# The first units of an attention stage: stacked operands of head 0 copied by engines, loads on two queues, the scale folded into a split, eight PSUM banks

## The chip, the core and the metric

The kernel runs on one core of a Trainium2 chip. The metric is the device time of one execution in microseconds (us). The engines are TensorE (PE, with its weight loads PEld), VectorE (DVE), ScalarE (ACT), GpSimd (POOL) and SyncE (SP). SP does no arithmetic; it issues DMA transfers, and so can ACT. SBUF is the on-chip memory of 128 partitions, PSUM the accumulator memory of eight banks.

## What is computed

```python
def _attn_ref(q, k, v, proj):            # 2 x 8 heads, 768 rows, 64 columns; proj 64 x 6
    scale = 1.0 / np.sqrt(D)
    q_bits = (einsum('bhsd,dk->bhsk', q, proj) > 0); k_bits = (... k ...)
    mask = q_bucket[..., :, None] == k_bucket[..., None, :]     # the six bits as one number
    scores = np.where(mask, scale * np.matmul(q, k.transpose(0, 1, 3, 2)), -1e9)
    attn = softmax over the last axis (denominator + 1e-9)
    return attn @ v
def reference(...):
    x = attention output as 1536 rows x 512
    x = _moe_ref(x, ...)      # router with noise, 2 of 8 experts, 512 -> 1024 -> 512, relu
    return _moe2_ref(x, ...)  # 512 -> 2048 -> 512 with h * sigmoid(1.702 h)
```

## The kernel before

The kernel is written engine by engine; each engine's program is a list in its own order, and semaphores order the engines among each other. Attention comes first, then the router, the experts and the last layer.

Attention works on 8 pairs of heads (PAIRS) and, for each head, on 6 blocks of 128 query rows; one block of one head is a step n, 96 steps in all. A step n is: `scores(n)` on TensorE into a psS bank pair, `statistics(n)` on VectorE (row maximum, and from it exp_arg), `exponentials(n)` on ACT, `transposes(n)` on TensorE into psT, `evac(n)` on ACT. The loop runs scores two steps ahead. `weighted` and `back` form the product with v for the head before.

A score is one product of stacked operands. A head's slot in W holds four tiles of 128 rows by 768 columns, QA, QB, KA and KB. QA is q_hi over q_hi, KA is k_hi over k_lo; QB is q_lo over the query's hash bits, and KB is k_hi over the key's hash bits. q_hi and q_lo are the two parts into which a float32 number is split for the fast product type (fp32r). So QA'KA + QB'KB gives the score and a large term that marks whether the hash bits agree.

A pair is prepared in eight units. Units 0 to 3 transpose q (0, 1) and k (2, 3), half of the columns each, for both heads at once (head 0 in partitions 0 to 63, head 1 in 64 to 127). ACT then copies the transposed half from PSUM into q_hi or k_hi, and VectorE subtracts it to form q_lo or k_lo. Units 4 to 7 multiply q and k by the hash matrices hash_m, and VectorE turns the result into bits (L938, one operation for each head and unit), which it writes straight into rows 64 to 127 of QB and KB. The remaining 12 pieces of 64 rows (6 of them q, 6 k) are moved from q_hi, q_lo, k_hi, k_lo into the slots by DMA from SP's queue (L420). For pair 0 all eight units run ahead of the first scores and use the four psS banks (`unit_bank`); for later pairs unit u of pair pr + 1 goes with step u of pair pr and uses psM.

The factor 1/8 is applied by POOL to the loaded q (L486) before the transposes; TensorE's unit 0 waits for it (`s_scaled`). POOL's list between two pairs also has `split_chunk(0, pr)`, which splits one of the first expert's weight chunks (L478, L480) once it has been staged:

```python
for pr in range(PAIRS):
    pool.wait_ge(s_q, 32 * (pr + 1))
    nc.gpsimd.tensor_scalar(q_raw[:], q_raw[:], SCALE, None, ALU.mult).then_inc(s_scaled, 1)
    if pr < 4:
        split_chunk(0, pr)
```

SP's list: q and k of pair 0 (L370), proj, the router's weights and the noise (L405 to L409); then for each pair the 12 stack moves, q and k of the next pair, v of this pair (L375), and a weight chunk (L381). VectorE first builds hash_m from proj (L907 to L920).

## Time and profile before

| what | value |
|---|---|
| median of 3 runs | 972.48 us (972.25 to 973.07) |
| the profiled execution: its own time | 973.35 us |
| its span in the trace | 971.6 us |
| TensorE busy | 893.4 us, 92% of the span |
| VectorE, ACT, POOL busy | 401.8, 402.5, 314.8 us |
| mean granted TensorE clock | 0.97 of full speed |
| attention, 0 to 302 us | TensorE busy 260.9 us |

Times in the trace are microseconds from the start of the span. Busy time is the time in which an engine had an instruction in work; the chain of waits is followed back from the last instruction, at each step to what released it. A granted clock of 1.00 is 2.4 GHz and 0.50 is 1.2 GHz. PEld, the weight load, overlaps PE.

### The profile page before, as it was taken

To read this page: it belongs to the slowest core of one execution; us is meant where nothing else is said; L and a number is where in the kernel's file an instruction comes from. 1 tells how busy PE (TensorE), PEld (TensorE's weight loads), DVE (VectorE), ACT (ScalarE), POOL (GpSimd) and SP (SyncE) were. 2 spreads that over 40 slices of the span, in tenths; PEclk is the share of its full clock that TensorE was granted. 3 is DMA by queue.
4 is the path that set the end of the run, shared out by engine and by line. 5 is a ranking of instruction groups with operands and counts; after the bars stand their busy time and mean duration, and the time that the engine had idled before them with its cause. 6 is when DMAs were issued, how large, how long until landed. Compare 5 with 4: busy or idle time off the path is not lost.

```text
span 971.6 us, 13442 instructions
## 1 busy us (share of the span) xinstructions
PE 893.4 (92%) x4964; PEld 779.9 (80%) x4964; DVE 401.8 (41%) x746; ACT 402.5 (41%) x687; POOL 314.8 (32%) x199
## 2 busy tenths in 40 slices
PE   3699999999998799999999999993699999999997
PEld 2566676666665689999999999993699999999996
DVE  4577767766774612222222222211443333333322
ACT  1566676676674124343343343411222322332222
POOL 1222020000240135564655656597970010000000
PEclk8899999999999789999999999998799999999999
DMA  7445624642423123655546456455331010000000
GB/s 161 112 115 152 163 71 104 168 115 57 110 89 109 29 64 124 184 160 177 165 158 192 161 163 196 147 181 170 127 95 38 32 43 22 32 0 0 33 1 32
DMA packets 66778, 103.34 MB, mean 106 GB/s; under 512 B 31676, under 2 KB 33724, under 8 KB 66716
## 3 DMA queue, kind: packets, MB, share of 16 engines
q1 hardware_dynamic: 55216, 76.65, 27.9%
q0 software_dynamic: 4480, 13.11, 4.5%
q10 hardware_dynamic: 7020, 12.78, 3.7%
q8 instruction: 36, 0.59, 0.3%
q14 instruction: 26, 0.21, 0.1%
HBM read 64.57 MB, written 19.07 MB: 86 GB/s over the span
## 4 chain that ended last, share of the span: by engine, by line
PE 82%; DVE 8%; issue 3%; ACT 2%; DMA 2%; SPq 2%; POOL 1%; ACTq 0%; DVEq 0%; POOLq 0%
PE psS L770 15%; PE psS L869 14%; PE psS L884 9%; PE psS L788 7%; PE psV L656 6%; PE psT L642 5%; PE psS L631 5%; PE psV L884 5%; PE psV L788 4%; PE psM L788 4%; DVE W L938 2%; PE psM L618 2%; PE psT L801 1%; ACT probT L1240 1%; PE psM L613 1%
## 5 line engine op out<-in xcount | busy, mean ns | idle before, releaser
L480 POOL TENSOR_TENSOR W<-staged,W 128x1024 fp32r<-128x1024 f32 x80 | 191.8, 2401 | 122.8 <-ACT W L1300 117.6
L770 PE MATMUL psS<-xT_hi,W 128*128 128x416 f32 x512 | 142.2, 359 | 1.1 <-DVE xT_lo L1113 1.1
L869 PE MATMUL psS<-x2T_hi,W 128*128 (+1 forms) x512 | 134.5, 344 | 1.6 <-DVE x2T_lo L1180 1.6
L1231 ACT ACTIVATE prob<-psS,exp_arg 128x768 f32<-128x768 f32 x96 | 95.5, 994 | 37.2 <-DVE exp_arg L947 37.1
L944 DVE TENSOR_REDUCE neg_max<-psS 128x1 f32<-128x768 f32 x96 | 91.5, 953 | 45.8 <-PE psS L631 44.9
L631 PE MATMUL psS<-W 128*128 128x384 f32 x384 | 93.8, 367 | 11.4 <-DMA W<-k_hi 9.4
L1240 ACT ACTIVATE probT<-psT 128x768 f32<-128x768 f32 x96 | 78.0, 812 | 57.8 <-PE psT L642 56.1
L869 PEld LDWEIGHTS psS<-x2T_hi,W 128*128 128x128 f32 x512 | 95.1, 192 | 6.8 <-issue 2.0
L1119 DVE SCALAR_TENSOR_TENSOR hT_lo<-psS,hT_hi 128x416 fp32r<-128x416 f32 x64 | 37.9, 591 | 149.5 <-ACT hT_hi L1293 132.0
L631 PEld LDWEIGHTS psS<-W 128*128 128x128 f32 x384 | 65.1, 194 | 38.6 <-issue 34.2
L770 PEld LDWEIGHTS psS<-xT_hi,W 128*128 128x128 f32 x512 | 92.7, 188 | 2.2 <-issue 1.2
L1187 DVE TENSOR_TENSOR g_sb<-psS,sig 128x384 f32<-128x384 f32 x64 | 35.7, 557 | 138.5 <-ACT sig L1374 138.5
L1374 ACT ACTIVATE sig<-psS 128x384 f32<-128x384 f32 x64 | 31.4, 491 | 146.0 <-PE psS L869 146.0
L770 PE MATMUL psS<-xT_lo,W 128*128 128x416 f32 x256 | 89.9, 351 | 0.0
L478 POOL TENSOR_TENSOR W<-staged,ones_col 128x1024 fp32r<-128x1024 f32 x24 | 45.8, 1909 | 134.5 <-DMA staged<-in_moe_w 96.0
L869 PE MATMUL psS<-x2T_lo,W 128*128 (+1 forms) x256 | 87.6, 342 | 0.0
L642 PE MATMUL psT<-ident,prob 128*128 128x128 f32 x576 | 80.0, 275 | 5.6 <-ACT probT L1240 5.6
L884 PE MATMUL psS<-W,g_hi 128*128 128x512 f32 x256 | 79.9, 393 | 1.7 <-issue 1.7
L642 PEld LDWEIGHTS psT<-ident,prob 128*128 128x128 f32 x576 | 66.8, 142 | 16.3 <-issue 13.1
L1300 ACT ACTIVATE W<-staged 128x1024 fp32r<-128x1024 f32 x56 | 59.1, 1055 | 30.6 <-DVE x_sb L1134 21.1
L788 PE MATMUL psS<-hT_hi,W 128*128 128x416 f32 x256 | 69.4, 352 | 0.0
L656 PE MATMUL psV<-probT,v_raw 128*64 128x384 f32 x360 | 68.0, 499 | 0.0
(221 smaller groups left out, 1397.4 us busy)
## 6 DMA issues: line engine op xcount, KB each, us to landing
staged<-in_moe_w SPq DMA_DIRECT2D x64, 512.0 KB
ys_dram<-x_sb ACTq DMA_DIRECT2D x60, 208.0 KB
W<-q_hi SPq DMA_DIRECT2D x32, 192.0 KB, 3.3
W<-k_hi SPq DMA_DIRECT2D x32, 192.0 KB, 3.7
staged<-in_moe_w_in SPq DMA_DIRECT2D x8, 512.0 KB
staged<-in_moe_w_out SPq DMA_DIRECT2D x8, 512.0 KB
q_raw<-in_q SPq DMA_DIRECT2D x16, 192.0 KB, 4.0
k_raw<-in_k SPq DMA_DIRECT2D x16, 192.0 KB, 4.2
```

The costliest lines, as they stand in the source:

```text
L480: nc.gpsimd.tensor_tensor(W[:, at + BLOCK:at + BLOCK + CH], staged[:, n % 2], W[:, at:at + CH].bitcast(F32), ALU.subtract).then_inc(s_spli ...
L631: last = nc.tensor.matmul(psS[:, n % 2, half, 0:HALF], stack(slot, a)[:, qt * P:(qt + 1) * P], stack(slot, b_)[:, half * HALF:(half + 1) * ...
L642: last = nc.tensor.transpose(psT[:, half, j * P:(j + 1) * P], prob[:, n % 2, c * P:(c + 1) * P], ident[:])
L656: last = nc.tensor.matmul(av_bank(hd)[half * D:(half + 1) * D, 0:HALF], v_raw[:, hd // 2 % 2, hd % 2, c * D:(c + 1) * D], probT[:, hd % 2, ...
L770: mm = nc.tensor.matmul(psS[:, 0, f % 2, 0:TM], W[:, at:at + P], x[:, t % 2, c], start=c == 0 and n == 0, stop=c == DC - 1 and n == 2)
L788: mm = nc.tensor.matmul(y_bank[d][:, 0:TM], W[:, at:at + P], h[:, f % 2], start=f == 0 and n == 0, stop=f == FC - 1 and n == 2)
L869: mm = nc.tensor.matmul(psS[:, 0, f % 2, 0:GN], W[:, at:at + P], x[:, bass.ds(buf + c * GN, GN)], start=c == 0 and n == 0, stop=c == DC - ...
L884: mm = nc.tensor.matmul(out_bank[j], gp[:, f % 2, j * P:(j + 1) * P], W[:, at:at + DM], start=f == 0 and n == 0, stop=f == GC - 1 and n == 2)
L944: nc.vector.tensor_reduce(neg_max[:, o, 0:1], psS[:, o, :, 0:HALF], mybir.AxisListType.XY, ALU.max, negate=True).then_inc(s_stat, 1)
L1231: nc.scalar.activation(prob[:, o, :].rearrange("p (a c) -> p a c", a=2), psS[:, o, :, 0:HALF], ACT.Exp, bias=exp_arg[:, o, 0:1], scale=exp ...
L1240: nc.scalar.activation(probT[:, hd % 2, :, t * P:(t + 1) * P].rearrange("p (a c) q -> p a c q", a=2), psT[:, :, 0:HALF].rearrange("p a (c ...
L1300: A(W[:, at:at + CH], staged[:, n % 2], ACT.Copy).then_inc(s_whi, 1)
```

## The change

For pair 0 alone, head 0's six stack pieces are written by engines in place of DMA: POOL copies q_hi twice into QA, VectorE copies q_lo into QB, ACT copies k_hi into KA and KB and k_lo into KA. Head 1's six pieces stay with SP, and `moved(pr)` counts the moves that are due (48 for pair 0, 96 for each later pair). `s_first` counts the six copies; `s_thr` counts the four threshold operations of head 0, which VectorE does first; those of head 1 follow between the first statistics. `scores(0)` waits for `s_first` and `s_thr` only, `scores(6)` for head 1's moves, and `transposes(0)` for all eight units, since units 4 to 7 of pair 0 now use psT, psV and psM.

The second head's q and k of pair 0 and the second half of proj are loaded from ACT's queue. SP loads q and k of pair 1 directly behind proj, ahead of the stack moves, and the router's weights and the noise behind v. POOL's scaling of q is gone for all pairs: ACT's q_hi is formed with scale 1/8 and VectorE's q_lo as PSUM times 1/8 minus q_hi. TensorE runs six products of ident with itself into psM before unit 0 (`unread(6)`), whose result nobody reads.

```diff
--- before.py
+++ after.py
@@ -216,7 +216,11 @@
 
         def unit_bank(u, first):
 
-            return psS[:, u // 2 % 2, u % 2] if first else psM
+            return (psS[:, 0, 0], psS[:, 0, 1], psS[:, 1, 0], psS[:, 1, 1], psT[:, 0], psT[:, 1], psV, psM)[u] if first else psM
+
+        def moved(pr):
+
+            return max(96 * pr - 48, 0)
 
         def columns(t, buf, j):
 
@@ -253,7 +257,8 @@
         s_den = sem("s_den")
         s_oT = sem("s_oT")
         s_back = sem("s_back")
-        s_scaled = sem("s_scaled")
+        s_first = sem("s_first")
+        s_thr = sem("s_thr")
         s_norm = sem("s_norm")
         s_x = sem("s_x")
 
@@ -355,8 +360,10 @@
             eng.wait_ge(s_exp, STEPS)
             eng.wait_ge(s_bias, STEPS)
             eng.wait_ge(s_back, HEADS)
-            eng.wait_ge(s_stq, 96 * PAIRS)
-            eng.wait_ge(s_stk, 96 * PAIRS)
+            eng.wait_ge(s_stq, moved(PAIRS))
+            eng.wait_ge(s_stk, moved(PAIRS))
+            eng.wait_ge(s_first, 6)
+            eng.wait_ge(s_thr, 4)
             eng.wait_ge(s_norm, HEADS)
 
         @block.sync
@@ -401,26 +408,30 @@
                     sp.wait_ge(s_osplit, 8 * (t - E + 1))
                     stage_over(t + 1, used)
 
-            load_qk(0)
+            sp.dma_start(q_raw[:, :, 0], q_v[0].rearrange("p (t d) -> p t d", d=D)).then_inc(s_q, 16)
+            sp.dma_start(k_raw[:, :, 0], k_v[0].rearrange("p (t d) -> p t d", d=D)).then_inc(s_k, 16)
             sp.dma_start(proj_sb[0:D, :], proj).then_inc(s_proj, 16)
-            sp.dma_start(proj_sb[D:P, :], proj).then_inc(s_proj, 16)
-            sp.dma_start(w_router[:, :, 0:E], w_gate.rearrange("(c p) e -> p c e", p=P)).then_inc(s_wr, 16)
-            sp.dma_start(w_router[:, :, E:2 * E], w_noise.rearrange("(c p) e -> p c e", p=P)).then_inc(s_wr, 16)
-            sp.dma_start(noise_sb[:].rearrange("p (b t) e -> p b (t e)", b=B),
-                         noise.rearrange("(b p t) e -> p b (t e)", b=B, t=NT)).then_inc(s_wr, 16)
+            load_qk(1)
             for pr in range(PAIRS):
                 if pr >= 2:
                     sp.wait_ge(s_S, PS * (pr - 1))
                 for hi, lo, s, u in ((q_hi, q_lo, s_stq, 2), (k_hi, k_lo, s_stk, 4)):
                     sp.wait_ge(s_ud, UNITS * pr + u)
-                    for hh in range(2):
+                    for hh in range(0 if pr else 1, 2):
                         rows, slot = slice(hh * D, (hh + 1) * D), 2 * (pr % 2) + hh
                         moves = (((QA, 0, hi), (QA, 1, hi), (QB, 0, lo)), ((KA, 0, hi), (KA, 1, lo), (KB, 0, hi)))[u // 2 - 1]
                         for which, at, src in moves:
                             sp.dma_start(stack(slot, which)[at * D:(at + 1) * D].bitcast(F32), src[rows].bitcast(F32)).then_inc(s, 16)
-                if pr + 1 < PAIRS:
+                if pr == 0:
+                    load_v(0)
+                    sp.dma_start(w_router[:, :, 0:E], w_gate.rearrange("(c p) e -> p c e", p=P)).then_inc(s_wr, 16)
+                    sp.dma_start(w_router[:, :, E:2 * E], w_noise.rearrange("(c p) e -> p c e", p=P)).then_inc(s_wr, 16)
+                    sp.dma_start(noise_sb[:].rearrange("p (b t) e -> p b (t e)", b=B),
+                                 noise.rearrange("(b p t) e -> p b (t e)", b=B, t=NT)).then_inc(s_wr, 16)
+                elif pr + 1 < PAIRS:
                     load_qk(pr + 1)
-                load_v(pr)
+                if pr:
+                    load_v(pr)
                 if pr < 6:
                     stage_chunk(0, pr)
             for c in range(6, 8):
@@ -481,11 +492,12 @@
                                         ALU.subtract).then_inc(s_split, 1)
 
             pool.wait_ge(s_const, 16)
-            for pr in range(PAIRS):
-                pool.wait_ge(s_q, 32 * (pr + 1))
-                nc.gpsimd.tensor_scalar(q_raw[:], q_raw[:], SCALE, None, ALU.mult).then_inc(s_scaled, 1)
-                if pr < 4:
-                    split_chunk(0, pr)
+            pool.wait_ge(s_hi, 2)
+            for which, at in ((QA, 0), (QA, 1)):
+                nc.gpsimd.tensor_scalar(stack(0, which)[at * D:(at + 1) * D], q_hi[0:D], 1.0, None, ALU.mult).then_inc(s_first, 1)
+            pool.wait_ge(s_first, 6)
+            for c in range(4):
+                split_chunk(0, c)
             pool.wait_ge(s_S, PS * (PAIRS - 1))
             for c in range(4, 8):
                 split_chunk(0, c)
@@ -595,15 +607,15 @@
             def unit(pr, u, first=False):
 
                 if u == 0:
-                    pe.wait_ge(s_scaled, pr + 1)
+                    pe.wait_ge(s_q, 32 * (pr + 1))
                 if u == 2:
                     pe.wait_ge(s_k, 32 * (pr + 1))
                 if u == 4 and first:
                     pe.wait_ge(s_hash, 18)
                 if not first:
                     pe.wait_ge(s_ud, UNITS * pr + u)
-                elif u >= 4:
-                    pe.wait_ge(s_ud, u - 3)
+                elif u in (4, 6):
+                    pe.wait_ge(s_ud, u - 2)
                 side, half = (u // 2) % 2, u % 2
                 ps = unit_bank(u, first)
                 if u < 4:
@@ -621,10 +633,13 @@
             def scores(n):
 
                 slot, qt = (n // NT) % 4, n % NT
-                if n % PS == 0:
+                if n == 0:
+                    pe.wait_ge(s_thr, 4)
+                    pe.wait_ge(s_first, 6)
+                elif n == NT or n % PS == 0:
                     pe.wait_ge(s_ud, UNITS * (n // PS + 1))
-                    pe.wait_ge(s_stq, 96 * (n // PS + 1))
-                    pe.wait_ge(s_stk, 96 * (n // PS + 1))
+                    pe.wait_ge(s_stq, moved(n // PS + 1))
+                    pe.wait_ge(s_stk, moved(n // PS + 1))
                 at_least(pe, s_exp, n - 1)
                 for i, (a, b_) in enumerate(((QA, KA), (QB, KB))):
                     for half in range(2):
@@ -636,6 +651,8 @@
             def transposes(n):
                 pe.wait_ge(s_exp, n + 1)
                 at_least(pe, s_evA, n)
+                if n == 0:
+                    pe.wait_ge(s_ud, UNITS)
                 for half in range(2):
                     for j in range(NT // 2):
                         c = half * (NT // 2) + j
@@ -665,7 +682,13 @@
                     last = nc.tensor.transpose(av_bank(hd)[:, j * P:(j + 1) * P], oT(hd)[:, j * P:(j + 1) * P], ident[:])
                 last.then_inc(s_back, 1)
 
+            def unread(n):
+
+                for i in range(n):
+                    nc.tensor.matmul(psM[:, 0:P], ident[:], ident[:], start=True, stop=True)
+
             pe.wait_ge(s_const, 8)
+            unread(6)
             for u in range(UNITS):
                 unit(0, u, True)
             for n in range(2):
@@ -919,13 +942,16 @@
                         nc.vector.tensor_scalar(hash_m[rows, side, m, cols[0]], src[rows], size, None, ALU.mult).then_inc(s_hash, 1)
                         nc.vector.tensor_scalar(hash_m[rows, side, m, cols[1]], src[rows], -size, None, ALU.mult).then_inc(s_hash, 1)
 
-            def unit(pr, u, first=False):
+            def unit(pr, u, first=False, heads=(0, 1)):
                 ps = unit_bank(u, first)
                 if u < 4:
                     c = slice((u % 2) * HALF, (u % 2 + 1) * HALF)
                     dve.wait_ge(s_hi, 4 * pr + u + 1)
                     hi, lo = ((q_hi, q_lo), (k_hi, k_lo))[u // 2]
-                    last = nc.vector.tensor_tensor(lo[:, c], ps[:, 0:HALF], hi[:, c].bitcast(F32), ALU.subtract)
+                    if u < 2:
+                        last = nc.vector.scalar_tensor_tensor(lo[:, c], ps[:, 0:HALF], SCALE, hi[:, c].bitcast(F32), ALU.mult, ALU.subtract)
+                    else:
+                        last = nc.vector.tensor_tensor(lo[:, c], ps[:, 0:HALF], hi[:, c].bitcast(F32), ALU.subtract)
                 else:
                     side, half = (u // 2) % 2, u % 2
                     c = slice(half * HALF, (half + 1) * HALF)
@@ -933,10 +959,10 @@
                     if u == 4:
                         at_least(dve, s_S, PS * (pr - 1))
                     t, s, w = ((thrQ, sclQ, QB), (thrK, sclK, KB))[side]
-                    for hh in range(2):
+                    for hh in heads:
                         rows = slice(hh * D, (hh + 1) * D)
                         last = nc.vector.tensor_scalar(stack(2 * (pr % 2) + hh, w)[D:P, c], ps[rows, 0:HALF], t[rows], s[rows], ALU.is_gt, ALU.mult)
-                last.then_inc(s_ud, 1)
+                last.then_inc(s_ud if 1 in heads else s_thr, 1)
 
             def statistics(n):
                 o = n % 2
@@ -965,10 +991,17 @@
                                         row_rec[:, hd % 2].rearrange("p (a j) -> p a j", a=2)[:, :, :, None].to_broadcast([P, 2, NT // 2, D]),
                                         ALU.mult).then_inc(s_norm, 1)
 
-            for u in range(UNITS):
+            for u in range(4):
                 unit(0, u, True)
+                if u == 1:
+                    dve.wait_ge(s_ud, 2)
+                    nc.vector.tensor_copy(stack(0, QB)[0:D], q_lo[0:D].bitcast(F32)).then_inc(s_first, 1)
+            for u in range(4, UNITS):
+                unit(0, u, True, (0,))
             for n in range(2):
                 statistics(n)
+                for u in (2 * n + 4, 2 * n + 5):
+                    unit(0, u, True, (1,))
             for n in range(STEPS):
                 hd, t = divmod(n, NT)
                 if t == 0 and hd >= 2:
@@ -1221,8 +1254,10 @@
                 c = slice((u % 2) * HALF, (u % 2 + 1) * HALF)
                 act.wait_ge(s_unit, UNITS * pr + u + 1)
                 if u in (0, 2) and not first:
-                    act.wait_ge((s_stq, s_stk)[u // 2], 96 * pr)
-                nc.scalar.activation((q_hi, k_hi)[u // 2][:, c], unit_bank(u, first)[:, 0:HALF], ACT.Copy).then_inc(s_hi, 1)
+                    act.wait_ge((s_stq, s_stk)[u // 2], moved(pr))
+                    act.wait_ge(s_first, 6)
+                nc.scalar.activation((q_hi, k_hi)[u // 2][:, c], unit_bank(u, first)[:, 0:HALF], ACT.Copy,
+                                     scale=SCALE if u < 2 else 1.0).then_inc(s_hi, 1)
 
             def exponentials(n):
                 o = n % 2
@@ -1240,8 +1275,15 @@
                 nc.scalar.activation(probT[:, hd % 2, :, t * P:(t + 1) * P].rearrange("p (a c) q -> p a c q", a=2),
                                      psT[:, :, 0:HALF].rearrange("p a (c q) -> p a c q", q=P), ACT.Copy).then_inc(s_evA, 1)
 
+            act.dma_start(q_raw[:, :, 1], q_v[1].rearrange("p (t d) -> p t d", d=D)).then_inc(s_q, 16)
+            act.dma_start(k_raw[:, :, 1], k_v[1].rearrange("p (t d) -> p t d", d=D)).then_inc(s_k, 16)
+            act.dma_start(proj_sb[D:P, :], proj).then_inc(s_proj, 16)
             for u in range(4):
                 unit(0, u, True)
+            act.wait_ge(s_hi, 4)
+            for which, at, src, done in ((KA, 0, k_hi, 0), (KB, 0, k_hi, 0), (KA, 1, k_lo, 4)):
+                at_least(act, s_ud, done)
+                nc.scalar.activation(stack(0, which)[at * D:(at + 1) * D], src[0:D].bitcast(F32), ACT.Copy).then_inc(s_first, 1)
             exponentials(0)
             for n in range(STEPS):
                 if n + 1 < STEPS:
```

## Rows read from the trace of the kernel before

**Rows 1.** The page's chain that ended last: shares of the span by engine.

```profile
PE 82%; DVE 8%; issue 3%; ACT 2%; DMA 2%; SPq 2%; POOL 1%; ACTq 0%; DVEq 0%; POOLq 0%
```

**Rows 2.** Table of stages: length, then each engine's busy us, clock, DMA share, GB/s.

```profile
0.00:302.00 302.00, 260.86 (x1584) 187.01 (x1584) 202.54 (x370) 186.64 (x321) 53.36 (x44) 0.97 0.45 114
302.00:345.00 43.00, 34.75 (x202) 30.08 (x203) 24.73 (x93) 12.68 (x22) 6.50 (x15) 0.82 0.24 82
```

**Rows 3.** Chain of waits, first 60 us: start, length, what.

```profile
18.37 0.67 SPq L420
...
23.66 4.52 DMA staged<-in_moe_w
...
28.25 1.90 POOL W L478
...
30.23 2.34 POOL W L480
32.56 2.10 POOL q_raw L486
...
34.71 0.90 PE psM L613 x3
```

**Rows 4.** Timeline, first 50 us: start, length, engine, line, operation.

```profile
0.82 1.28 ACT L1225 ACT_TABLE_LOAD   x1 [0.82 <-PEq L1418]
...
5.26 2.16 POOL L486 TENSOR_SCALAR q_raw<-q_raw 128x768 f32<-128x768 f32 x1 [1.63 <-DMA q_raw<-in_q]
...
6.90 0.55 DVE L907 CAST proj_hi<-proj_sb 128x6 fp32r<-128x6 f32 x1 [6.90 <-DMA proj_sb<-in_proj]
...
7.57 1.51 PE L613 MATMUL psS<-ident,q_raw 128*128 128x128 f32 x6 [7.57 <-POOL q_raw L486]
...
9.11 1.08 DVE L928 TENSOR_TENSOR q_lo<-psS,q_hi 128x384 fp32r<-128x384 f32 x2
9.12 0.49 ACT L1225 ACTIVATE q_hi<-psS 128x384 fp32r<-128x384 f32 x1
...
11.51 5.58 DVE L938 TENSOR_SCALAR W<-psS,thr 64x384 fp32r<-64x384 f32 x8
...
22.60 2.90 PE L631 MATMUL psS<-W 128*128 128x384 f32 x8 [9.38 <-DMA W<-k_hi]
...
24.26 0.96 DVE L944 TENSOR_REDUCE neg_max<-psS 128x1 f32<-128x768 f32 x1 [7.17 <-PE psS L631]
25.25 0.16 DVE L947 SCALAR_TENSOR_TENSOR exp_arg<-neg_max 128x2 f32<-128x2 f32 x1
...
27.39 0.82 PE L642 MATMUL psT<-ident,prob 128*128 128x128 f32 x6
...
35.65 0.49 ACT L1225 ACTIVATE q_hi<-psM 128x384 fp32r<-128x384 f32 x1 [6.59 <-PE psM L613]
...
36.69 1.48 PE L642 MATMUL psT<-ident,prob 128*128 128x128 f32 x6
...
42.68 0.97 PE L631 MATMUL psS<-W 128*128 128x384 f32 x4
```

**Rows 5.** Short stretches: columns as in rows 2, after the length.

```profile
4.50:5.00 0.50, 0.00 (x0) 0.00 (x0) 0.00 (x0) 0.00 (x0) 0.00 (x0) 1.00 1.26 284
...
34.00:35.00 1.00, 0.29 (x2) 0.29 (x3) 0.00 (x0) 0.00 (x0) 0.66 (x1) 0.50 0.00 0
```

**Rows 6.** DMA issues of the first 8 us: KB each, median us to landing.

```profile
q_raw<-in_q SPq DMA_DIRECT2D x2, 192.0 KB, 3.3
k_raw<-in_k SPq DMA_DIRECT2D x2, 192.0 KB, 3.5
...
proj_sb<-in_proj SPq DMA_DIRECT2D x2, 1.5 KB, 2.5
```

**Rows 7.** Timeline of a weight chunk's split.

```profile
61.03 2.13 DVE L947 SCALAR_TENSOR_TENSOR exp_arg<-neg_max 128x2 f32<-128x2 f32 x1
```

**Rows 8.** Groups of VectorE, 0 to 310: count, busy us, mean ns.

```profile
L947 DVE SCALAR_TENSOR_TENSOR exp_arg<-neg_max 128x2 f32<-128x2 f32 x96 | 26.3, 274 | 3.3
```

## The prediction

> **What bounds the kernel now.** I began with the page. Its chain of waits runs through TensorE for 82% of the span [rows 1], so a change pays only where TensorE stands still. The table of stages gives attention 302 us, with TensorE busy for 260.9 of them, and the routing stage behind it 43 us [rows 2]. The diff touches the first unit of work of head 0, the q scaling in front of every pair, and nothing past attention; so I read attention's first 43 us.
>
> The chain of waits [rows 3] shows two holes. First: SP issues the twelve stack transfers one after another; the last issue ends at 19.04 (18.37 + 0.67) and the first score product starts at 22.60 [rows 4]. TensorE stood still for 9.4 us before it. Second: after the first transposes of probabilities (27.39 + 0.82 = 28.2) TensorE stands still until 34.71 [rows 3, 4]. It waits for pair 1's q to be scaled by POOL, and POOL sits in program order behind weight chunk 0, whose transfer lands at 28.2, plus 1.90 and 2.34 us of split and 2.10 us of scaling [rows 3]. The reader is to see that the second hole hangs on SP's queue too: chunk 0 is issued behind all stack transfers, pair 1's q and k, and v. From 35.65, where ACT evacuates the first q unit of pair 1 [rows 4], the steps follow one another without such holes. So I use the start of that q_hi, 35.65, as the milestone: behind it both kernels have the same order of work, and what the milestone gains the end gains, unless something takes it back.
>
> **The change, part by part, up to the first scores.**
>
> *Loads on two queues.* Landing takes 3.3 us for q, 3.5 for k, 2.5 for proj [rows 6]. The queues begin at 0.8, as ACT's table load does [rows 4]; q was landed when POOL took it at 5.26. With the second half issued beside the first, q lands at 0.8 + 3.3 = 4.1 at the earliest. If ACT's first issue stands behind its table load (0.82, 1.28 us [rows 4]) it lands near 2.1 + 3.3 = 5.4. I take 4.7. The DMA engines are already full at 284 GB/s in 4.5 to 5.0 [rows 5], and the four loads are 768 KB, so k cannot land much before 5.5, and proj, behind it, lands near 5.8 instead of 6.8. The six products of unread() start once ident is there and are six transposes long, 1.5 us at the pace of the first ones [rows 4]; they end before q lands and cost nothing. With a q that landed at once they would cost up to 1.5.
>
> *No scaling by POOL before the transposes.* POOL's 2.16 us (5.26 to 7.42 [rows 4]) leaves the path. From the first q transpose to the end of the second q_hi took 9.12 + 0.49 - 7.57 = 2.04 us, so both q_hi halves stand at 4.7 + 2.1 = 6.8. The factor inside the split is one more operand of an operation of 384 columns: nothing, on ACT and on DVE. At worst it is 0.05 us each.
>
> *VectorE becomes the path.* It builds the hash matrices: 6.90 to 9.11 now, of which the first cast took 0.55 us and ended at 7.45, as POOL's scaling ended (7.42) [rows 4]; a small one takes 0.16, so it lost about 0.4. From 5.8 that is 1.8 us: done at 7.6. Then q_lo, two for 1.08; the new copy of q_lo, 64 rows by 768; k_lo, 1.1; and four threshold operations of head 0 alone, where eight took 5.58, so 2.8. The copy is not in the trace: a reduction over 768 columns takes 0.96 [rows 4], a small operation like exp_arg 0.16 [rows 4], and I take 0.6. Sum 1.1 + 0.6 + 1.1 + 2.8 + 0.15 of handovers = 5.75, so scores could start at 13.4.
>
> *POOL's new copies against VectorE.* POOL copies q_hi twice, 64 rows by 768. Its scaling of 768 columns took 2.16; I take that for each, so POOL is busy about 4.3 us from 6.8, before score operands are due. But the first cast above waited for POOL's end, and an exp_arg of 0.16 us took 2.13 us while POOL split a chunk [rows 7]. VectorE's hash operations (5.8 to 7.6) and its q_lo copy read and write SBUF like that cast. They can lose from nothing to 4.3 us, the first scores then starting at 13.4 or 17.7. The two meet for certain, by these times, and half of the work would be caught: I take 2.2, scores at 15.6. The Trainium skill ("SBUF — State Buffer", Who interferes with whom) says the pair of ports is locked for a whole instruction, and that whichever of the two engines issues first blocks the other. By it the bound is one POOL copy caught at a time: 15.5 if one catches VectorE, 17.7 if both do; the cast's row agrees.
>
> *Copies on ACT.* Three of 768 columns; q_hi of 384 takes 0.49 [rows 4], so 0.98 each. Two run behind k_hi (near 8.5 to 10.4) and the third behind k_lo, beside the 2.8 us of thresholds. Cost nothing; without that cover 1.
>
> *Twelve stack transfers less six.* Head 0 needs none. Head 1's six are issued between roughly 10 and 18 and land, at the 4.5 us of the weight chunk [rows 3], by 22.5. Its first scores are step 6, now at 42.68 [rows 4], then at about 32: hidden.
>
> **From the first scores to the milestone.** Scores to first reduction takes 24.26 - 22.60 = 1.66. VectorE then does statistics (0.96 + 0.16 + handovers, 1.2), two thresholds of head 1 (1.4), statistics (1.2), two thresholds (1.4): 5.2. This is a wait that before had not: the transposes of step 0 now write psT, from which unit 5's thresholds are read last, and wait for all eight units. Queued behind them are pair 1's first unit, and ACT's evacuation. Then transposes take 0.82, or 1.48 at the lower clock (0.50 granted in 34 to 35 [rows 5]), and unit 0 of pair 1 to q_hi 0.94 (35.65 - 34.71), or about 0.65 at the higher. The whole is 9.3 at the low and about 7.7 at the high one. TensorE is idle for under 3 us here instead of 6.5; I take 8.6. The milestone: 15.6 + 8.6 = 24.2, against 35.65: 11.4 us.
>
> The second hole is thereby gone: POOL no longer stands between q and its transposes. Pair 1's q and k are issued once the first transposes are done, about 6.3 to 9, and landed long before 22. What is late next is VectorE, not a transfer.
>
> **What takes some back.** Weight chunk 0 is split now in the hole, 28.25 to 32.56, where nobody cares. Afterwards its transfer, issued near 17 to 20, lands 4.5 us later [rows 3], and the 4.2 us of split falls on steps 0 to 2. An exp_arg caught loses up to 1.97 [rows 7]; two can be caught, and some of it lies under ACT's other work. I charge 0.7 (0 to 4). The seven later scalings on POOL cost the path nothing, since no transpose waited for them; their going gives nothing. The same chunks 1 to 7 meet the same steps, shifted; their collisions may change by 1 each way.
>
> Sum: 973.35 (the profiled execution, span 971.6) - 11.4 + 0.7 = 962.7. It lies 0.9 above the median of the runs, 972.48; so 961.8.
>
> Bounds. Best: scores at 13.4, milestone 7.7 later, nothing taken back: 35.65 - 21.1 = 14.6, time 957.9. Worst: 17.7 and 9.3, 4 taken back: 35.65 - 27.0 - 4 = 4.6, time 967.8. Not all bad ends meet, so 957.5 to 966.5.
>
> **Rivals.**
>
> *Part of the gain goes to the lock between VectorE and POOL.* Both copies catch VectorE fully and chunk 0 catches two exp_args that all count: the worst above, 965 to 968. For it: rows 7 and the cast. Against: ACT's work covers some of it.
>
> *Slower: the lock in the steps.* All exp_args together lost 26.3 - 96 x 0.16 = 10.9 us to it [rows 8], at most about 2 each. The eight chunks bring 16 POOL operations; if every one caught one exp_arg fully, each losing the length of its split less 0.16 [rows 3, 4], that is 8 x 1.7 + 8 x 2.2 = 31 us, 20 more than now, and 973.35 - 11.4 + 20 - 0.9 = 981. It decides from six more full catches on. Against: chunks 4 to 7 are released by a step's scores, so they meet the same exp_args as now.
>
> *Same: the transfers give it back.* If head 1's operands landed only when they are needed today (42.7), 11 us late for the new step 6, nothing would be left: 972.5. For it: they now share the DMA engines with pair 1's loads. Against: 20 us of room.
>
> *More than the sum.* VectorE is not caught, and TensorE keeps its clock: the best above, 956 to 958.
>
> **How the numbers follow.** The forecast (957.5 to 965) 0.76; most lost to the lock (965 to 970.5) 0.13; more than the sum 0.05; given back 0.03; slower 0.03. A measurement here can tell 0.2%, 1.9 us. The first three are faster: 0.94; same 0.03; slower 0.03.
>
> **What would show it.** The first score product near 15.6, and no DMA in front of it but VectorE's threshold. Transposes of step 0 released by VectorE near 22 to 23; ACT's first q_hi from psM near 24. No wait of TensorE for q_raw or POOL. VectorE's hash operations or its q_lo copy far longer than 0.16 and 0.6 while POOL copies: the lock, and how much. Exp_arg near 2 us in steps 0 to 3. Attention's end near 291. Wrong it would be if ACT's loads came late by its table load beyond 1.3 us, if POOL's copies take far over 2.2 us each, or if a later stage holds work that waits for a time and not for a step.

## The result, and the profile after

The changed kernel takes 961.05 us (median of 4 runs, 959.97 to 961.26), against 972.78 for the kernel before: ratio 0.9872, 95% interval 0.9855 to 0.989. The forecast was 961.8, between 957.5 and 966.5. The profiled execution takes 960.99 with a span of 959.1, so 12.4 and 12.5 us less than that of before. By the medians it is 972.78 - 961.05 = 11.7 us.

The page's chain and the table of stages of the changed kernel, to be held against [rows 1, 2]:

```profile
PE 83%; DVE 9%; issue 3%; ACT 2%; DMA 2%; POOL 1%; SPq 0%; ACTq 0%; DVEq 0%; POOLq 0%
```

```profile
0.00:290.00 290.00, 262.92 (x1599) 188.04 (x1600) 204.81 (x371) 188.70 (x324) 41.35 (x40) 0.99 0.46 115
```

Attention is over some 12.5 us earlier. The timeline of its first 30 us (start, length, engine, line, operation, and in brackets the idle time before it and its releaser), against [rows 4]:

```profile
2.24 2.93 PE L688 MATMUL psM<-ident 128*128 128x128 f32 x12 [2.24 <-POOL ident L469]
...
4.96 1.49 PE L625 MATMUL psS<-ident,q_raw 128*128 128x128 f32 x6
...
6.59 0.17 DVE L930 CAST proj_hi<-proj_sb 128x6 fp32r<-128x6 f32 x1 [6.59 <-DMA proj_sb<-in_proj]
...
7.15 4.62 POOL L497 TENSOR_SCALAR W<-q_hi 64x768 fp32r<-64x768 f32 x2 [3.53 <-ACT q_hi L1259]
...
7.22 0.80 DVE L943 TENSOR_SCALAR hash_m<-proj_hi 64x6 fp32r<-64x6 f32 x1
...
8.56 0.80 DVE L943 TENSOR_SCALAR hash_m<-proj_hi 64x6 fp32r<-64x6 f32 x1
...
9.48 1.02 DVE L952 SCALAR_TENSOR_TENSOR q_lo<-psS,q_hi 128x384 fp32r<-128x384 f32 x2
...
10.54 0.55 DVE L998 CAST W<-q_lo 64x768 fp32r<-64x768 f32 x1
...
12.95 0.67 DVE L964 TENSOR_SCALAR W<-psT,thr 64x384 fp32r<-64x384 f32 x1 [0.22 <-PE psT L630]
...
13.91 0.67 DVE L964 TENSOR_SCALAR W<-psV,thr 64x384 fp32r<-64x384 f32 x1 [0.29 <-PE psV L630]
...
14.51 0.66 DVE L964 TENSOR_SCALAR W<-psM,thr 64x384 fp32r<-64x384 f32 x1
...
15.22 1.67 PE L646 MATMUL psS<-W 128*128 128x384 f32 x8 [0.78 <-DVE W L964]
...
21.35 1.51 PE L659 MATMUL psT<-ident,prob 128*128 128x128 f32 x6 [1.83 <-DVE W L964]
22.06 1.89 POOL L489 TENSOR_TENSOR W<-staged,ones_col 128x1024 fp32r<-128x1024 f32 x1 [10.28 <-DMA staged<-in_moe_w]
22.23 1.73 DVE L973 SCALAR_TENSOR_TENSOR exp_arg<-neg_max 128x2 f32<-128x2 f32 x1
...
23.61 0.48 ACT L1259 ACTIVATE q_hi<-psM 128x384 fp32r<-128x384 f32 x1
...
25.58 0.85 DVE L973 SCALAR_TENSOR_TENSOR exp_arg<-neg_max 128x2 f32<-128x2 f32 x1
...
27.60 0.97 PE L646 MATMUL psS<-W 128*128 128x384 f32 x4
```

The reader is to see four things. The scores start at 15.22 in place of 22.60, released by VectorE's threshold (the bracket) and no longer by a transfer. The transposes of step 0 wait for VectorE at 21.35. The first q_hi of pair 1 starts at 23.61 in place of 35.65, 12.04 earlier, and nothing waits for POOL there. And VectorE is caught: hash operations of 0.16 us take 0.80 while POOL copies, exp_arg takes 1.73 and 0.85 while POOL splits chunk 0 (0.16 otherwise).

Where the gain stands as the steps go on is read from the starts of ACT's evacuations (L1240 before, L1275 after), which both kernels have in the same order. The table gives how many us earlier than in the kernel before each of them starts, for the changed kernel, for a second profile of the same kernel, and for the experiments below.

| kernel | q_hi of pair 1 | step 4 | step 32 | step 36 | step 92 |
|---|---|---|---|---|---|
| changed | 12.04 | 13.03 | 13.24 | 12.56 | 12.64 |
| changed, again | 11.10 | 11.55 | 11.55 | 11.57 | 11.66 |
| scale in the split alone | 5.66 | 5.84 | 6.36 | 6.07 | 6.11 |
| head 0 by DMA | 4.43 | 4.74 | 5.20 | 5.05 | 5.02 |
| all loads on SP | 10.93 | 11.36 | 11.83 | 11.85 | 11.87 |
| no unread | 11.38 | 12.26 | 12.75 | 12.78 | 12.76 |
| POOL after the hash matrices | 13.69 | 12.93 | 13.25 | 13.25 | 13.33 |
| split with one input | 12.50 | 11.98 | 12.41 | 12.41 | 12.85 |
| all thresholds first | 10.41 | 11.34 | 11.76 | 11.81 | 11.74 |
| no lock, no-match left out | 12.09 | 12.09 | 12.54 | 12.55 | 13.42 |
| no lock, exact | 12.91 | 14.10 | 14.20 | 14.10 | 14.73 |
| the same, gaps filled | 13.38 | 14.84 | 14.89 | 14.95 | 15.54 |
| the same, gaps idle | 11.40 | 12.86 | 12.70 | 12.75 | 13.58 |

Behind attention the programs are the same, but not their times: from POOL's first gather to the end of the span it is 638.0 us before, 638.2 after, 637.2 in the second profile, and from 635.1 (all loads on SP) to 639.2 (split with one input) in the others. So an edit worth less than 2 us is not read from the whole time, but from this table. Each row is one profile, and the two rows of the changed kernel differ by 0.9 to 1.7 us, so the table doesn't tell differences of that size either, unless the rows of the trace show where they come from.

### The profile page after: what moved, and what is told of

Its sections match the earlier page's. It is cut to its first block, busy times and chain, and to the rows that moved or that the text cites. A ratio compares the mean times of both kernels' runs of the same rounds, so it can differ in the third digit from the quotient of the medians.

```text
span 959.1 us, 13465 instructions
## 1 busy us (share of the span) xinstructions
PE 895.8 (93%) x4976; PEld 780.6 (81%) x4976; DVE 403.6 (42%) x747; ACT 405.0 (42%) x690; POOL 302.7 (32%) x193
## 4 chain that ended last, share of the span: by engine, by line
PE 83%; DVE 9%; issue 3%; ACT 2%; DMA 2%; POOL 1%; SPq 0%; ACTq 0%; DVEq 0%; POOLq 0%
PE psS L793 15%; PE psS L892 14%; PE psS L907 9%; PE psS L811 7%; PE psV L673 6%; PE psS L646 5%; PE psV L907 5%; PE psT L659 5%; PE psV L811 4%; PE psM L811 4%; DVE W L964 3%; PE psM L630 2%; PE psT L824 1%; DVE neg_max L970 1%; ACT probT L1275 1%
## 5 line engine op out<-in xcount | busy, mean ns | idle before, releaser
L1275 ACT ACTIVATE probT<-psT 128x768 f32<-128x768 f32 x96 | 78.0, 812 | 57.5 <-PE psT L659 55.7
L646 PE MATMUL psS<-W 128*128 128x384 f32 x384 | 91.6, 360 | 3.9 <-ACT prob L1266 3.0
```

The costliest lines, as they stand in the source:

```text
L646: last = nc.tensor.matmul(psS[:, n % 2, half, 0:HALF], stack(slot, a)[:, qt * P:(qt + 1) * P], stack(slot, b_)[:, half * HALF:(half + 1) * ...
L1275: nc.scalar.activation(probT[:, hd % 2, :, t * P:(t + 1) * P].rearrange("p (a c) q -> p a c q", a=2), psT[:, :, 0:HALF].rearrange("p a (c ...
```

## The experiments

**1. The second hole alone.** The kernel before, with only the scaling moved.

```diff
-                    pe.wait_ge(s_scaled, pr + 1)
+                    pe.wait_ge(s_q, 32 * (pr + 1))
...
-                pool.wait_ge(s_q, 32 * (pr + 1))
-                nc.gpsimd.tensor_scalar(q_raw[:], q_raw[:], SCALE, None, ALU.mult).then_inc(s_scaled, 1)
```

with ACT's scale and VectorE's factor as in the change. 

> The kernel before, with one part of the change alone: the factor 1/8 inside the split of q, and no scaling by POOL for any pair. Theory (two holes, each removed by its own part): the second hole of 6.5 us goes, since pair 1's transposes wait for the load alone, and the first cast no longer stands behind POOL (0.4); the exp_arg of step 2, held by chunk 0's split until 30.2, now counts, up to 0.8. First scores at 22.2, ACT's first q_hi from psM at 29 to 30 in place of 35.65; 966.5, between 965 and 968. Rival (one chain: the new transposes just wait longer for something else, such as pair 1's q, issued behind the stack moves and landing near 25, or chunk 0's split on VectorE): gain under 4 us, above 968.5.

966.24 us, ratio 0.9912 (0.9892 to 0.9933). First scores at 22.34, q_hi at 29.99. The second hole was worth 6.1 us by itself at step 92, and the rival falls. The whole time fell by more, 8.6 us against the 974.88 that the kernel before took on the same chip; 1.8 of that lies behind attention in the profile (636.2 in place of 638.0), where nothing was edited. So the milestone confirms the theory, and the hit on 966.5 is in part chance.

**2. The first hole put back.** The changed kernel with head 0's pieces moved by SP.

```diff
-            return max(96 * pr - 48, 0)
+            return 96 * pr
...
-                    for hh in range(0 if pr else 1, 2):
+                    for hh in range(2):
...
-            for which, at in ((QA, 0), (QA, 1)):
-                nc.gpsimd.tensor_scalar(stack(0, which)[at * D:(at + 1) * D], q_hi[0:D], 1.0, None, ALU.mult).then_inc(s_first, 1)
```

and the same for VectorE's and ACT's copies; scores(0) waits for the moves. 

> The changed kernel, with head 0's six stack pieces moved by SP's DMA again; all else stays. Theory: the engine copies carry the first hole. SP's twelve moves are issued from 10 to 19 and landed near 22, so scores start near 21.5 to 22.5 in place of 15.2, and ACT's first q_hi from psM comes near 30 in place of 23.6; 967, between 966 and 968.5. Rival (the copies only move the wait: thresholds and statistics on VectorE fill the time either way, since the milestone waits for all eight units): the milestone moves by under 3 us, below 964.

968.87 us, ratio 0.9938 (0.9918 to 0.9958), 0.4 above the expected range, and q_hi at 31.22 where 30 was expected. The timeline of this run:

```profile
6.55 0.17 DVE L926 CAST proj_hi<-proj_sb 128x6 fp32r<-128x6 f32 x1 [6.55 <-DMA proj_sb<-in_proj]
...
8.39 1.02 DVE L948 SCALAR_TENSOR_TENSOR q_lo<-psS,q_hi 128x384 fp32r<-128x384 f32 x2
...
22.18 2.90 PE L642 MATMUL psS<-W 128*128 128x384 f32 x8 [8.74 <-DMA W<-k_hi]
...
28.96 1.51 PE L655 MATMUL psT<-ident,prob 128*128 128x128 f32 x6 [1.16 <-DVE W L960]
...
31.22 0.49 ACT L1251 ACTIVATE q_hi<-psM 128x384 fp32r<-128x384 f32 x1
```

Scores are back at 22.18, and by the table the engine copies are worth 12.64 - 5.02 = 7.6 us, or 6.6 against the second profile. This kernel has everything else of the change and is yet 1.1 slower at step 92 than experiment 1: its transposes of step 0 wait for head 1's thresholds (28.96). So with head 0 moved by DMA the rest of the change (queues, order of loads, banks, thresholds, unread) brings nothing beyond experiment 1 that shows. The engine copies are priced here with the second hole gone; no run has them alone on the kernel before. The run also prices the lock: without POOL's copies the time from the cast to q_lo is 8.39 - 6.55 = 1.84 us, with them 9.48 - 6.59 = 2.89. VectorE lost 1.05. In three other kernels without POOL's copies at that time (experiments 1, 6 and 12) this stretch is 1.84 too.

**3. One queue.** The three loads of ACT's queue moved back to SP's, in the old order.

```diff
-            act.dma_start(q_raw[:, :, 1], q_v[1].rearrange("p (t d) -> p t d", d=D)).then_inc(s_q, 16)
-            act.dma_start(k_raw[:, :, 1], k_v[1].rearrange("p (t d) -> p t d", d=D)).then_inc(s_k, 16)
-            act.dma_start(proj_sb[D:P, :], proj).then_inc(s_proj, 16)
```

> The changed kernel, with all six loads of pair 0 issued by SP again, in the old order. Theory: the second queue saves issue time only, of which the bytes hide part: proj lands near 6.9 in place of 6.5, q near 5.2 in place of 4.8. POOL then starts near 7.5, and its catch of VectorE stays. First scores 0.3 to 0.8 us later, time up by 0.3 to 0.8. Rival (the queues moved nothing, because the DMA engines are full): no change within 0.2. Second rival (proj late and POOL late no longer overlap as now, the catch changes): up by 1 to 2.

961.48 us, ratio 0.9863 (0.9842 to 0.9883). First scores at 15.64, 0.42 later than in the first profile of the changed kernel and 0.16 later than in the second. The transposes of q started at the same time (4.97), and proj came 0.34 and 0.49 later (6.93); but q_lo started only 0.05 and 0.16 later (9.53), since VectorE was held for less while POOL copied. The same program up to the first scores gave them at 14.76 in experiment 7. So what the second queue is worth, under half a microsecond, is lost in the spread, and the run tells neither the theory nor the rival.

**4. No unread products at the start.**

```diff
-            unread(6)
```

> The changed kernel without the six unread products ahead of the first unit. They took 2.93 us in the trace and ended about when q landed. Theory 1: they buy a higher TensorE clock earlier: without them the k transposes and the hash products up to 14.3 run at the lower pace, first scores 0.3 to 0.6 us later, time up by 0.3 to 1. Theory 2: nothing waits for TensorE there, VectorE being the path: no change within 0.3, or down by 0.1.

961.04 us, ratio 0.9858 (0.9838 to 0.9878). First scores at 15.21, as in the changed kernel, and the first transposes at 4.98, released by the load of q, so the unread products hold nothing up; but the eight of them take 2.93 us and not 1.67, and q_hi comes at 24.27. That looked like theory 1, until the kernel was run again.

**5. The changed kernel again.** No edit. 

> The changed kernel again, unaltered, to see what of the differences between runs lies in the chip and not in the edit. Theory (the moment at which TensorE's clock rises again near 24 us is not set by the kernel): first scores at 15.2 and ACT's first q_hi from psM near 23.6 come back within 0.1, but the evacuation of step 4, 31.51 in the first run, comes between 31.5 and 32.6, since two other runs that are the same kernel up to there gave 32.45 and 32.56. Time 960 to 962. Rival (it repeats): 31.5 within 0.1.

961.22 us (960.54 to 964.28), ratio 0.9877 (0.985 to 0.9904). Its timeline, and the stretches of both profiles (length, busy us of PE, PEld, DVE, ACT and POOL, then the granted clock), the first profile first:

```profile
15.48 2.93 PE L646 MATMUL psS<-W 128*128 128x384 f32 x8 [0.77 <-DVE W L964]
...
22.29 1.51 PE L659 MATMUL psT<-ident,prob 128*128 128x128 f32 x6 [1.16 <-DVE W L964]
...
24.55 0.48 ACT L1259 ACTIVATE q_hi<-psM 128x384 fp32r<-128x384 f32 x1
```

```profile
15.00:17.00 2.00, 1.67 (x8) 1.35 (x8) 0.93 (x2) 0.00 (x0) 0.00 (x0) 1.00 0.99 207
17.00:21.00 4.00, 0.97 (x4) 0.65 (x4) 3.83 (x8) 2.16 (x4) 0.00 (x0) 0.96 1.01 244
21.00:26.00 5.00, 4.65 (x26) 4.54 (x26) 4.74 (x6) 2.97 (x7) 3.87 (x2) 0.69 0.05 19
```

```profile
15.00:17.00 2.00, 1.52 (x5) 1.52 (x6) 0.42 (x1) 0.00 (x0) 0.00 (x0) 0.50 1.01 207
17.00:21.00 4.00, 2.92 (x9) 2.04 (x7) 3.67 (x7) 1.22 (x3) 0.00 (x0) 0.50 0.98 241
21.00:26.00 5.00, 3.84 (x17) 3.64 (x17) 3.95 (x6) 3.10 (x6) 3.60 (x2) 0.50 0.04 15
```

The same program got a clock of 1.00 for its first scores once and 0.50 the other time. Six unread products at 2.2 us do not settle that: of the seven profiles that have them and in which TensorE idled for some 0.8 us before the first scores, five got 1.00 (the first, and experiments 6, 7, 9 and 10) and two 0.50 (this one and experiment 3); without them, in one profile, it was 0.50. The step-4 entry differs by 1.5 us between two profiles of one kernel, and at step 92 1.0 is left; 0.7 of it went between steps 32 and 36, where the first profile had an exp_arg of 2.31 us and the second two of 0.63 and 1.27:

```profile
111.02 2.31 DVE L973 SCALAR_TENSOR_TENSOR exp_arg<-neg_max 128x2 f32<-128x2 f32 x1
```

So the kernel does not repeat, and the rival falls. The theory was too narrow: first scores came 0.26 and q_hi 0.94 later, not within 0.1, and step 4 at 32.99, not by 32.6.

**6. POOL's copies later.** One wait more, in POOL's list.

```diff
             pool.wait_ge(s_hi, 2)
+            pool.wait_ge(s_hash, 18)
```

> The changed kernel, with one more wait: POOL starts its two copies of q_hi only when VectorE has built the hash matrices. Theory (the two engines' common lock costs VectorE 1.1 us: hash matrices done at 9.4 in place of 8.3): first scores at 14.1 to 14.3 in place of 15.22, time 1.0 lower, 960. POOL's copies end near 13.1, before the last threshold. Rival (the catch only moves to the q_lo copy, which then wants its 0.55 us inside POOL's first copy): first scores 14.9 or later, gain under 0.4. Second rival (TensorE's earlier start falls into the stretch at the lower clock, 10.7 to 13.6): the first scores come earlier but run at the lower pace, gain 0.4 to 0.7.

960.66 us, ratio 0.9872 (0.9857 to 0.9887).

```profile
8.50 4.37 POOL L498 TENSOR_SCALAR W<-q_hi 64x768 fp32r<-64x768 f32 x2 [4.88 <-DVE hash_m L944]
...
9.38 0.55 DVE L999 CAST W<-q_lo 64x768 fp32r<-64x768 f32 x1
...
13.97 1.67 PE L647 MATMUL psS<-W 128*128 128x384 f32 x8 [0.76 <-DVE W L965]
...
21.96 0.48 ACT L1260 ACTIVATE q_hi<-psM 128x384 fp32r<-128x384 f32 x1
...
24.15 2.37 POOL L491 TENSOR_TENSOR W<-staged,W 128x1024 fp32r<-128x1024 f32 x1
24.17 2.37 DVE L974 SCALAR_TENSOR_TENSOR exp_arg<-neg_max 128x2 f32<-128x2 f32 x1
```

The scores start at 13.97, 1.25 and 1.51 earlier than in the two profiles of the changed kernel (0.79 than in experiment 7, the same program up to there), so the lock's price of 1.05 came back. They ran at the higher pace (1.67), so the second rival falls too. The cast of q_lo took 0.55 inside POOL's first copy: it was not held, and the first rival falls. But the 1.65 won at q_hi (21.96) was gone at step 4: an exp_arg met the second half of chunk 0's split at its first moment and lost 2.2. What remained at step 92 is 13.33, against 12.64 and 11.66.

**7. The chunk's first half with one input.**

```diff
-                    nc.gpsimd.tensor_tensor(W[:, at:at + CH], staged[:, n % 2], ones_col[:].to_broadcast([P, CH]), ALU.mult).then_inc(s_whi, 1)
+                    nc.gpsimd.tensor_scalar(W[:, at:at + CH], staged[:, n % 2], 1.0, None, ALU.mult).then_inc(s_whi, 1)
```

> The changed kernel, with the first half of POOL's chunk split (128 x 1024, a product with a broadcast column of ones) written as a product with the constant 1.0, one tensor input. Theory (what holds exp_arg is a two-input operation on POOL; in the trace of before an exp_arg at 64.06 ran in 0.16 inside POOL's scaling): no exp_arg is held by this half; it takes 2.8 in place of 1.9 us. All exp_args together lose 8 to 10 us in place of 12.3, and time falls by 1 to 2. Rival (the lock is the same for every POOL operation that reads SBUF): the half is longer, so the loss grows, 13 to 17 us, and time rises by 0.5 to 3.

961.74 us, ratio 0.9879 (0.9864 to 0.9895).

```profile
110.59 2.77 POOL L489 TENSOR_SCALAR W<-staged 128x1024 fp32r<-128x1024 f32 x1 [28.36 <-DMA staged<-in_moe_w]
...
111.85 0.16 DVE L973 SCALAR_TENSOR_TENSOR exp_arg<-neg_max 128x2 f32<-128x2 f32 x1
```

An exp_arg, with its two inputs in SBUF, ran in 0.16 us in the middle of POOL's operation with one input. In this profile nine exp_args start inside that operation, and all nine took 0.16; six start inside the split's second half, which still has two inputs, and all six ended with it (0.81 to 2.35 us). Over all 96 the loss fell to 23.1 - 96 x 0.16 = 7.7 us (12.3 in the changed kernel, 10.4 in its second profile), a little less than the 8 to 10 expected. From step 8 to step 92 the gain grew by 0.85, where it fell by 0.4 in the changed kernel and grew by 0.1 in its second profile. The expected 1 to 2 us in the whole time did not show.

**8. All thresholds first.** Besides the lines below, scores(0) waits for all eight units.

```diff
-            for u in range(4, UNITS):
-                unit(0, u, True, (0,))
+            for u in range(4, UNITS):
+                unit(0, u, True)
             for n in range(2):
                 statistics(n)
-                for u in (2 * n + 4, 2 * n + 5):
-                    unit(0, u, True, (1,))
```

> The changed kernel, with both heads' thresholds ahead of the first scores, in the old order; banks, copies and loads stay. Scores start 2.6 to 2.8 us later, near 18.0. Theory (the milestone waits for all eight units either way): the transposes of step 0 then wait for the exponentials alone, near 18.0 + 1.0 + 1.2 + 1.2 = 21.4, where they are now at 21.35, and ACT's first q_hi from psM stays at 23.6 to 23.9; time within 0.3 of the changed kernel. Rival (doing head 0 first is worth its 2.7 us): milestone near 26, time up by 2 to 2.7.

960.24 us, ratio 0.9872 (0.9856 to 0.9889).

```profile
17.56 2.93 PE L645 MATMUL psS<-W 128*128 128x384 f32 x8 [3.33 <-DVE W L963]
...
23.02 1.48 PE L658 MATMUL psT<-ident,prob 128*128 128x128 f32 x6
...
25.24 0.49 ACT L1256 ACTIVATE q_hi<-psM 128x384 fp32r<-128x384 f32 x1
```

Scores 2.3 us later, q_hi 1.6 later than in the first profile of the changed kernel and 0.7 than in the second. At the low clock, which both had, this kernel and the second profile meet again: 11.34 and 11.55 at step 4, 11.74 and 11.66 at step 92. So head 0's thresholds first bring scores forward and the end by nothing that these runs tell; the theory holds at equal clock, its figure for q_hi does not.

**9. exp_arg without SBUF inputs.** The maximum goes to a spare PSUM column, and exp_arg is the smaller of it and the bound; rows without a matching key are not treated.

```diff
-                nc.vector.scalar_tensor_tensor(exp_arg[:, o], neg_max[:, o, 0:1].to_broadcast([P, 2]), NO_MATCH, neg_max[:, o],
-                                               ALU.is_lt, ALU.mult).then_inc(s_bias, 1)
+                nc.vector.tensor_scalar(exp_arg[:, o], pair, NO_MATCH, None, ALU.min).then_inc(s_bias, 1)
```

> The changed kernel, with the row maximum written to a spare PSUM column and exp_arg formed by one operation that reads PSUM alone: the smaller of the value and the bound. It leaves out the case of a row with no matching key, whose softmax is then not uniform. Theory (the lock in the steps is on the path): no exp_arg over 0.2 us, the 12.3 us that they lose in sum vanish, and of them some 5 to 8 lie on the path: 953 to 956. Rival (TensorE has slack in its queue there, or the next operation is caught instead, as row_den was for 2.3 us): under 2 us.

961.27 us, ratio 0.9873 (0.9852 to 0.9894). All 96 took 0.16, 15.3 us in sum. From step 8 (12.09) to step 92 (13.42) the gain grew by 1.33, against a loss of 0.41 (13.05 to 12.64) in the changed kernel, 1.7 us apart. But that profile is the extreme one: its second profile and experiments 3, 4, 6 and 8, which keep exp_arg as it was, grew by 0.12 to 0.51 over the same steps. So 0.8 to 1.7 us lay on the path, of some 10 to 12 lost in sum. The expected 953 to 956 was wrong. That TensorE had work queued behind most of the late exp_args would explain it; no run shows that.

**10. The same, exact, with POOL's copies later.** The bound is read from SBUF, the maximum as scalar operand; POOL's copies wait as in experiment 6. One line of the edit:

```diff
+                nc.vector.scalar_tensor_tensor(exp_arg[:, o], neg_max[:, 0], pair[:, 0:1], pair, ALU.is_gt, ALU.mult)
```

> The changed kernel with POOL's copies behind the hash matrices and exp_arg free of the lock, now with rows without a match treated as before: the bound from SBUF, the maximum as scalar operand and the pair from PSUM, one operation. Theory: first scores at 14.0, no exp_arg over 0.2, and from step 8 to step 92 1.7 us less than in the changed kernel, as in the run that left the no-match case out; attention ends 1.5 to 2.9 us earlier than in the changed kernel (evacuation of step 92 at 273.6 to 275.0 against 276.49), time 957.5 to 960. Rival (stalls of the path are rare and the rest is TensorE's own work): under 1.

958.79 us (958.29 to 959.72), ratio 0.9847 (0.9821 to 0.9872); the changed kernel on the same chip had 960.54 to 964.28, six executions each, so even the slowest of this kernel is below the fastest of that one. First scores at 14.21, each exp_arg 0.22, the evacuation of step 92 at 274.40, inside the expected range. From step 8 to step 92 the gain grew by 0.87: 1.3 us better than the first profile of the changed kernel and 0.75 than the second, not 1.7.

**11 and 12. The gaps of TensorE filled, and left idle.** On top of experiment 10, with all thresholds first; experiment 12 leaves the two added lines out.

```diff
+            unread(12, psS[:, 0, 1])
             for n in range(2):
                 scores(n)
+            unread(6)
```

> As the run before, with all thresholds ahead of the first scores and TensorE kept busy in its two gaps: twelve unread products of 128 columns between the last hash product and the first scores, six behind the second scores. Theory (the order of thresholds is worth nothing, the clock is worth 1 to 2 us): first scores near 16.5 at the higher pace (8 products in 1.7), transposes of step 0 near 20.8, ACT's first q_hi from psM at 21.5 to 22.3; evacuation of step 92 at 273 to 274.5; time 956.5 to 959. Rival (the unread products come in front of scores that were ready, or the clock falls all the same): q_hi at 23 or later, no better than the run before.

> The run before without its eighteen unread products in the two gaps; TensorE idles there, from about 12.9 to 16.5 and after the second scores. The six at the start stay. Theory (in that run the clock stayed at its higher level from 15 to 26 because of them, and that is what they are worth): first scores at 16.5 as before, but at the lower pace (8 products in 2.9), ACT's first q_hi from psM at 23.5 to 24.2 in place of 22.27, evacuation of step 4 at 31.2 to 32.2 in place of 29.70, and of step 92 1.5 to 2.5 later than 273.59. Rival (the gap is too short for the clock to fall): q_hi within 0.3 of 22.27.

958.59 us (956.49 to 960.87), ratio 0.9844 (0.9817 to 0.9871), with the gaps filled; 960.35, ratio 0.9869 (0.9852 to 0.9885), with the gaps idle. Timeline and stretches with filled gaps, and then the stretches with idle ones:

```profile
12.88 2.84 PE L688 MATMUL psS<-ident 128*128 128x128 f32 x24
...
16.48 1.66 PE L646 MATMUL psS<-W 128*128 128x384 f32 x8 [0.76 <-DVE W L966]
...
20.70 0.82 PE L659 MATMUL psT<-ident,prob 128*128 128x128 f32 x6
...
22.27 0.48 ACT L1261 ACTIVATE q_hi<-psM 128x384 fp32r<-128x384 f32 x1
```

```profile
17.00:21.00 4.00, 3.60 (x26) 3.37 (x25) 2.38 (x5) 2.17 (x4) 0.00 (x0) 1.00 0.78 205
21.00:26.00 5.00, 4.84 (x35) 3.94 (x34) 3.91 (x7) 4.44 (x9) 4.27 (x2) 1.00 0.00 0
```

```profile
17.00:21.00 4.00, 2.85 (x9) 2.34 (x8) 2.38 (x4) 1.35 (x3) 0.00 (x0) 0.50 0.79 227
21.00:26.00 5.00, 4.98 (x27) 4.50 (x27) 2.42 (x4) 3.26 (x7) 4.26 (x2) 0.73 0.00 0
```

Filled, the clock stayed at 1.00 from 17 to 26, q_hi came at 22.27 and step 92 15.54 us before the kernel before. Idle, the clock was at 0.50 from 17 to 21, q_hi came at 24.25. 2.0 us lie between them, at step 4 and still at step 92. Both came out as forecast (q_hi at 24.25 lies 0.05 above its range). But this is one profile of each, on two chips, of a thing that went both ways in two profiles of one program. The last three hash products took 0.34 us each from 12.36 on in the filled run, so its clock was up before the filling began; in the idle run they still took 0.52, and its clock was 1.00 in 15 to 16 and fell before 17. What speaks for the filling is that in the five profiles with a long stand of TensorE ahead of its first scores (the kernel before and experiments 1, 2, 8 and 12; 3.33 to 9.38 us) the eight products took 2.77 to 2.93 us. That the filling is worth 2.0 us is not shown.

On one chip the medians of experiments 10 and 11 lie 2.4 and 2.6 us below that of the changed kernel, and all executions of 10 and five of the six of 11 below its fastest. Between the two there are 0.2 us in the median, so the filled gaps with all thresholds first show no gain in time over experiment 10.

## Why the prediction was right, point by point

- **Two holes, and both go.** Right. Experiments 1 and 2 price them: 6.1 us for the second alone, 6.6 to 7.6 for the engine copies once the second is gone. Both releasers are as forecast: VectorE's threshold, and no load or POOL.
- **q and proj.** q landed for transposes at 4.96 (4.7 forecast). proj came at 6.59, not 5.8: its landing took 3.8 and 4.2 us behind the other loads, where I had only let it wait for the bytes. ACT's table load stood behind its issues (2.95) and cost nothing. What the second queue itself brings is not told (experiment 3).
- **unread costs nothing.** Right, though it took 2.93 us (2.24 to 5.17, two records for each product) and not 1.5: without it the transposes started at 4.98, with it at 4.96.
- **The lock.** Right in kind, too large: 1.05 us, 2.2 forecast (experiments 2 and 6). Two catches, each holding hash operations for about 0.65, of which 0.65 and 0.4 counted; not one whole copy; the cast of 0.55 was not caught. The stretch from q_lo to the scores took 5.74, forecast 5.75, though its thresholds waited 0.5 for hash products. First scores 15.22, forecast 15.6: that it came so near is in part luck, since the lock at 1.15 too much and proj at 0.8 too little cancel.
- **To the milestone.** 8.39 us, forecast 8.6. The new wait for all eight units is there (21.35). What I had not seen is that putting head 0's thresholds first is not what brings the gain (experiment 8). In the second profile the milestone came at 24.55, 9.07 after the scores.
- **What is taken back.** This term was mis-sized. I charged 0.7 from the milestone on. Two exp_args were caught as forecast (1.73 and 0.85), but the gain grew, by 1.0 to step 4 (0.45 in the second profile). The kernel before ran these steps at the lower clock after its hole [rows 4, 5], 0.50 up to 38 us and 0.69 in 38 to 40; the changed one, whose milestone is 12 us earlier, had 0.50 up to 24 and 0.98 in 24 to 26. That fits the growth; no run tests it alone. Later, near step 36, one exp_arg of 2.31 us took 0.7 back; "1 each way" held. In the sum, 10.7 us were forecast and 12.4 measured between the two profiles, 11.7 between the medians. Of the 1.7 between the profiles 0.6 were won up to the milestone and 1.3 behind it (0.7 not taken and 0.6 given), and 0.3 went behind attention; so the size of this term was wrong, and the total was saved by its being small.
- **The rivals.** Head 1's pieces came in time: its scores started at 27.60, and TensorE did not wait for them. The slower case was open only if all of exp_arg's loss lay on the path; experiment 9 puts 0.8 to 1.7 of 10 to 12 us there, so it was far off. The bounds were drawn by hand: the best case adds up to 957.9, while the last rival says 956 to 958, and the chances give the forecast 957.5 to 965 where the range goes to 966.5.

The Trainium skill ("SBUF — State Buffer", Who interferes with whom) says that a VectorE operation with two SBUF inputs contends with any GpSimd operation that reads SBUF. The trace of experiment 7 differs: while POOL's operation had one tensor input, nine of nine exp_args passed in 0.16 us; with two, six of six were held to its end, for up to 2.2 us more. Here the measurement decides. The two operations also differ in kind (tensor_scalar and tensor_tensor), and no run parts the kind from the number of inputs.

## What to carry to other kernels

When a list of transfers stands between two engines at the start, count its issues: twelve issues took 9 us, and engines that were idle did half of them in the shadow of other work. When two waits stand in series, price each alone, and after removing one look for the next that ends last. And before reading an edit of 1 us from a whole time, run the unaltered kernel twice and compare the same step in both traces; here one and the same kernel moved by 1.5 at step 4, at different clocks.

## What the runs showed of the hardware

- One program, two profiles, and TensorE's granted clock in 15 to 17 us was 1.00 and 0.50; scores took 1.67 and 2.93 us. With products that nobody reads in the gaps it stayed at 1.00 from 15 to 26, in one profile; what they are worth is not shown.
- VectorE's operations with one tensor input, both ends in SBUF (0.16 us), were held twice for about 0.65 us by a POOL copy of 2.2 us, the first time released in its middle (8.02, where the copy ran from 7.15 to 9.33); a cast of 0.55 us was not held (10.54), and in experiments 7 and 8 it took 0.90, after the second of the two catches had not come. When a catch comes was not found. In sum the catches cost 1.0 to 1.1 us in six profiles (the changed kernel twice, experiments 4, 7, 8 and 9) and 0.8 in experiment 3.
- exp_arg (two inputs in SBUF) that starts inside POOL's product or difference of two tensors is held to its end, up to 2.2 us more, and not by its scaling of one tensor (experiment 7). With one input in PSUM none of the 96 was held, and each took 0.22 in place of 0.16 (experiments 10 to 12).
